# Ranks ahead of half of G, an earlier row table, two gathers in flight, and two weight loads held back, in a fused attention and two-MoE kernel

## What is computed

```python
# soft MoE: 32 slots, 4 for each of 8 experts
c = softmax(x @ phi, axis=1)                   # N x 32
x = c @ slot_out                               # slot_out is 32 x 512
# top-2 MoE
noisy = x @ w_gate + log1p(exp(x @ w_noise)) * noise
top2, top2_w = two best experts of each token, softmax of their two scores
for e in range(8):
    for k in range(2):
        rows = top2[:, k] == e
        h = np.maximum(x[rows] @ w1[e], 0.0)
        out[rows] += top2_w[rows, k, None] * (h @ w2[e])
```

## Time and profile before

| | |
|---|---|
| Median of 3 runs | 1070.62 us (1070.4 to 1071.17) |
| Profiled execution, its own time | 1072.71 us |
| Its span | 1070.9 us |
| Busy share of the span | PE 90%, DVE 73%, POOL 58%, ACT 57% |
| Chain that ended last, by engine | PE 31%, DVE 28%, issue 23%, POOL 6%, DMA 6%, ACT 3% |
| Mean DMA traffic | 98 GB/s |

### The profile page before, as it was taken

The page is one execution under the profiler, slowest core; times in us unless marked ns, Lnnn a source line. Parts: engine busy times, 40 slices in busy tenths (PEclk is TensorE's granted clock), DMA queues, the critical chain, the costliest instruction groups (busy, mean ns, idle before and its releaser), DMA issues.

```text
span 1070.9 us, 21707 instructions
## 1 busy us (share of the span) xinstructions
PE 962.8 (90%) x6439; PEld 674.3 (63%) x6439; DVE 785.2 (73%) x1511; ACT 612.2 (57%) x1243; POOL 621.4 (58%) x940
## 2 busy tenths in 40 slices
PE   3899998999999999999999989997699999999995
PEld 1566666666666666666666676332377878777884
DVE  5999999999999999999999963105735443554251
ACT  2787887787778878778878872102323332333121
POOL 3577777777777777777777760001444544555453
PEclk9999999999999999999999999998899999999998
DMA  9910110110110010010010006899915534433332
GB/s 349 421 46 34 47 30 15 45 45 12 33 45 12 33 45 12 33 45 21 24 45 12 0 1 229 329 420 422 384 22 120 120 42 113 117 42 41 43 41 32
DMA packets 23776, 105.14 MB, mean 98 GB/s; under 512 B 3200, under 2 KB 4288, under 8 KB 16576
## 3 DMA queue, kind: packets, MB, share of 16 engines
q1 hardware_dynamic: 15856, 84.54, 20.6%
q0 software_dynamic: 7168, 11.21, 8.0%
q10 hardware_dynamic: 720, 8.98, 2.3%
HBM read 88.39 MB, written 16.07 MB: 98 GB/s over the span
## 4 chain that ended last, share of the span: by engine, by line
PE 31%; DVE 28%; issue 23%; POOL 6%; DMA 6%; ACT 3%; DVEq 1%; SPq 1%; POOLq 0%; ACTq 0%
PE psum L843 14%; DVE arena L1049 8%; PE psum L848 7%; DVE arena L1045 6%; DVE arena L1037 5%; DVE arena L1033 3%; POOL arena L1334 3%; DMA arena<-w_top 2%; ACT h_hi L1009 2%; DVE arena L1053 2%; DMA arena<-xs_rows,arena 2%; POOL arena L1371 2%; DVE arena L1041 2%; PE psum L830 1%; PE psum L719 1%
## 5 line engine op out<-in xcount | busy, mean ns | idle before, releaser
L1334 POOL TENSOR_SCALAR arena<-arena 128x576 bf16<-128x576 f32 x144 | 249.5, 1733 | 135.5 <-DVE arena L1033 128.5
L586 PE MATMUL psum<-arena 128*128 128x130 f32 (+3 forms) x1600 | 220.6, 279 | 2.8 <-ACT arena L891 2.8
L586 PEld LDWEIGHTS psum<-arena 128*128 128x128 f32 (+3 forms) x1600 | 185.6, 178 | 35.7 <-ACT arena L891 3.3
L543 PE MATMUL psum<-arena 64*128 64x288 f32 (+1 forms) x640 | 111.8, 462 | 58.1 <-DVE arena L1041 53.1
L1293 DVE COPY arena<-psum 128x512 f32 x41 | 28.3, 691 | 152.9 <-PE psum L848 120.5
L843 PE MATMUL psum<-w_hi,h_hi 128*128 128x512 f32 x320 | 131.4, 411 | 6.5 <-ACT h_hi L1009 1.8
L871 ACT ACTIVATE arena<-arena 128x576 bf16<-128x576 bf16 x144 | 98.6, 685 | 64.6 <-POOL arena L1334 64.5
L1009 ACT ACTIVATE h_hi<-psum 128x512 fp32r<-128x512 f32 x80 | 43.4, 595 | 160.3 <-PE psum L830 159.5
L843 PE MATMUL psum<-w_lo,h_hi 128*128 128x512 f32 x320 | 126.9, 396 | 0.0
L1037 DVE MAX8 arena<-psum 128x8 f32<-128x576 f32 x144 | 109.3, 759 | 14.4 <-PE psum L555 13.3
L865 ACT COPY arena<-psum 128x576 f32<-128x576 f32 x144 | 90.6, 629 | 38.4 <-PE psum L543 38.1
(11 more groups left out here) (198 smaller groups left out, 1629.2 us busy)
## 6 DMA issues: line engine op xcount, KB each, us to landing
weights<-w_soft SPq DMA_DIRECT2D x21, 1024.0 KB, 16.1
arena<-qkv SPq DMA_DIRECT2D x15, 864.0 KB, 4.4
weights<-w_top SPq DMA_DIRECT2D x12, 1024.0 KB, 25.9
arena<-w_soft SPq DMA_DIRECT2D x11, 1024.0 KB, 9.5
weights<-w_top SPq DMA_DIRECT2D x3, 2048.0 KB, 26.6
weights<-w_top ACTq DMA_DIRECT2D x3, 2048.0 KB, 7.9
arena<-qkv SPq DMA_DIRECT2D x16, 325.0 KB, 2.9
out<-arena SPq DMA_DIRECT2D x1, 4864.0 KB, 18.3
```

What stands on the lines that cost most here:

```text
L543: last = nc.tensor.matmul(bank(2 * (t % 2) + x, SH)[q0:q0 + rows, :], qT[u][half, w * P + q0:w * P + q0 + rows], kT[u][half, h * SH:(h + 1 ...
L586: last = nc.tensor.matmul(o_place(n, k)[0:rows, :], wT[0:kr, t % 2, kc, q0:q0 + rows], v_, start=(kc == 0), stop=(kc == KC - 1))
L1334: nc.gpsimd.tensor_scalar(hit[t % 2], s_sb[t % S_SLOTS], m8[t % S_SLOTS][:, 7:8], None, ALU.is_ge) \
```

## The change

- PE: the rank matmuls move ahead of `g_part(0, 1)`. Reading the bounds moves from ahead of the L804 matmuls into `g_part(1, 1)`, two loads ahead of each of its four steps. `g_stack(4)` and `g_stack(5)` move from ahead of the loop into it: `g_stack(e + 4)` now follows experts 0 to 3.
- ACT: the write of the row table is issued after `g_high(0, 0)`. `g_out` of experts 0 to 3 goes ahead of `w2_high(0, 0)`. `w2_high(0, 1)` goes to POOL, as a copy, and `w2_high(1, 0)` goes behind the tiles of expert 0.
- DVE: takes `hi_hot`'s picked half and `w2_low(0, 0)` over from POOL. `w2_low(0, 0)` goes ahead of `c_low(1)`.
- POOL: the first gather has a semaphore of its own (`x_first`), and the second is issued without a wait for the first.
- SP: w2 of experts 2 and 3 is loaded only when both first gathers have landed.

```diff
@@ SP @@
             sp.wait_ge(g_ps, 2)
             for e in range(4):
+                if e == 2:
+                    sp.wait_ge(x_first, 16)
+                    sp.wait_ge(x_ready, 16)
                 load_w2t(sp, e)
@@ PE @@
-            def g_part(g, x):
+            def g_part(g, x, bounds=None):
...
                 for c in range(DC):
+                    if bounds is not None:
+                        bounds += [tile_bound(pe, 2 * c + 1), tile_bound(pe, 2 * c + 2)]
...
             g_part(0, 0)
-            g_part(0, 1)
 
             pe.wait_ge(st, 9)
...
+            g_part(0, 1)
             g_part(1, 0)
-            pe.wait_ge(rt_ready, 1)
-            bounds = tile_bounds(pe)
...
-            g_part(1, 1)
+            pe.wait_ge(rt_ready, 1)
+            bounds = [0]
+            g_part(1, 1, bounds)
...
-            for e in range(4, 6):
-                g_stack(e)
-            pe.wait_ge(w_lo_first, 1)
+            pe.wait_ge(g_lo, 4)
...
-                if e in (1, 2):
-                    g_stack(e + 5)
+                if e < 4:
+                    g_stack(e + 4)
@@ ACT @@
             g_high(0, 0)
+            act.wait_ge(rows_set, 1)
+            act.dma_start(xs_dram[0:ROWS, :].rearrange("(p a) r -> p (a r)", a=PICKS),
+                          rows_f).then_inc(tabled, 16)
             g_high(0, 1)
...
             g_high(1, 1)
+            for e in range(4):
+                g_out(e)
             w2_high(0, 0)
-            g_out(0)
-            g_out(1)
...
             x_copy(0, x_ring[:, 0:SL])
-            g_out(2)
-            g_out(3)
             c_high(1)
-            w2_high(0, 1)
             x_copy(1, x_ring[:, SL:2 * SL])
-            w2_high(1, 0)
...
+                if e == 0:
+                    w2_high(1, 0)
                 if e < E - 1:
                     w2_high(e + 1, 1)
@@ DVE @@
+            dve.wait_ge(hot_set, 1)
+            nc.vector.tensor_tensor(hi_hot[:, :, 0, :], col_hot,
+                                    cst[:, C_PICK:C_PICK + PICKS].unsqueeze(2).broadcast_to([P, PICKS, COLS]),
+                                    ALU.mult).then_inc(hot_hi, 1)
...
+            w2_low(0, 0)
             c_low(1)
             w2_low(0, 1)
@@ POOL @@
-            for n in range(2):
-                fetch(nowx[n], n, 0, idx_x, n)
-                if n > 0:
-                    pool.wait_ge(x_ready, 16 * n)
-                gather(n)
-            pool.wait_ge(w_hi, 1)
-            nc.gpsimd.tensor_tensor(w2_lo[0][:, 0:FC // 2, :], w2t_of(0)[:, 0:FC // 2, :],
-                                    w2_hi[0][:, 0:FC // 2, :].bitcast(F32), ALU.subtract).then_inc(w_lo_first, 1)
+            fetch(nowx[0], 0, 0, idx_x, 0)
+            gather(0, x_first)
+            fetch(nowx[1], 1, 0, idx_x, 1)
+            gather(1)
+            pool.wait_ge(g_ps, 4)
+            pool.wait_ge(w2t_in[0], 16)
+            nc.gpsimd.tensor_copy(w2_hi[0][:, FC // 2:FC, :], w2t_of(0)[:, FC // 2:FC, :]).then_inc(w_hi_pool, 1)
```

More of the change, by code:

```diff
@@ L314, in build @@
         pick_set = sem("pick_set")
-        hot_set, hot_dve, hot_act, hot_pool = sem("hot_set"), sem("hot_dve"), sem("hot_act"), sem("hot_pool")
+        hot_set, hot_dve, hot_act, hot_hi = sem("hot_set"), sem("hot_dve"), sem("hot_act"), sem("hot_hi")
         gate_set = sem("gate_set")
@@ L321, in build @@
         w2t_in = [sem(f"w2_top{s}") for s in range(4)]
-        x_ready, x_c = sem("x_ready"), sem("x_copied")
+        x_first, x_ready, x_c = sem("x_first"), sem("x_ready"), sem("x_copied")
         f_t = sem("f_t")
@@ L327, in build @@
         f_h, f_hc, f_lo = sem("f_h"), sem("f_hc"), sem("f_lo")
-        w_hi, w_lo, w_lo_first = sem("w2_hi"), sem("w2_lo"), sem("w2_lo_first")
+        w_hi, w_lo, w_hi_pool = sem("w2_hi"), sem("w2_lo"), sem("w2_hi_pool")
         f_y, f_yc = sem("f_y"), sem("f_yc")
@@ L838, in _ @@
                         if f % 4 == 0:
-                            if 2 * e + f // 4 > 0:
-                                pe.wait_ge(w_lo, 2 * e + f // 4)
+                            pe.wait_ge(w_lo, 2 * e + f // 4 + 1)
                             pe.wait_ge(f_hc, 2 * i + f // 4 + 1)
@@ L989, in x_copy @@
             def x_copy(n, slot):
-                act.wait_ge(x_ready, 16 * n + 16)
+                act.wait_ge(*((x_first, 16) if isinstance(n, int) and n == 0 else (x_ready, 16 * n)))
                 nc.scalar.copy(x_cur.rearrange("p (r s) -> p r s", r=4),
@@ L1019, in _ @@
                     g_out(e + 4, 2)
-            hold(act, x_ready, 16 * bounds[E] + 48)
+            hold(act, x_ready, 16 * bounds[E] + 32)
             hold(act, x_c, bounds[E] + 2)
@@ L1260, in w2_low @@
                 f = n * FC // 2
-                dve.wait_ge(w_hi, 2 * e + n + 1)
+                dve.wait_ge(*((w_hi, 1) if (e, n) == (0, 0) else (w_hi_pool, 1) if e == 0 else (w_hi, 2 * e + n)))
                 nc.vector.tensor_tensor(w2_lo[e % 4][:, f:f + FC // 2, :], w2t_of(e % 4)[:, f:f + FC // 2, :],
@@ L1415, in fetch, with gather @@
                 hold(pool, ready, count + 1)
-            def gather(slot):
+            def gather(slot, landed=x_ready):
                 nc.gpsimd.indirect_dma_start(
                     x_ring[:, slot * SL:slot * SL + SL], None, xs_dram[:, :], bass.IndirectOffsetOnAxis(ap=nowx[slot], axis=0),
-                    bounds_check=ROWS + P - 1, oob_is_err=True).then_inc(x_ready, 16)
+                    bounds_check=ROWS + P - 1, oob_is_err=True).then_inc(landed, 16)
             pool.sem_inc(out_free, 3)
@@ L1426, in _ @@
             pool.wait_ge(tabled, 16)
[L1427 to L1434 removed]
+            fetch(nowx[0], 0, 0, idx_x, 0)
[5 more added lines that the diff above has]
+            nc.gpsimd.tensor_copy(w2_hi[0][:, FC // 2:FC, :], w2t_of(0)[:, FC // 2:FC, :]).then_inc(w_hi_pool, 1)
             for n in range(2, AHEAD):
                 pool.wait_ge(x_c, n - 1)
+                if n == 2:
+                    pool.wait_ge(x_first, 16)
                 fetch(nowx[n % 2], n, 0, idx_x, n)
[L1438 removed]
+                pool.wait_ge(x_ready, 16 * n - 16)
                 gather(n % 2)
@@ L1448, in _ @@
                     fetch(nowx[k], 2 * i + k + AHEAD, 0, idx_x, 2 * i + k + AHEAD)
-                    hold(pool, x_ready, 32 * i + 16 * k + 16 * AHEAD)
+                    hold(pool, x_ready, 32 * i + 16 * k + 16 * AHEAD - 16)
                     gather(k)
@@ L1452, in _ @@
                     pool.sem_inc(out_free, 1)
-            hold(pool, x_ready, 32 * pairs + 16 * AHEAD)
+            hold(pool, x_ready, 32 * pairs + 16 * AHEAD - 16)
 def constants():
```

10 lines of the change are left out of this document (1 added, 9 removed).

## The result

| | before | changed |
|---|---|---|
| Median (lowest to highest) | 1070.61 us (1069.68 to 1071.17, 5 runs) | 1075.91 us (1074.44 to 1076.93, 5 runs) |
| Ratio, 95% interval | | 1.0049 [1.0034, 1.0064] |
| Profiled execution, its own time | 1072.71 us | 1074.75 us |
| Its span | 1070.9 us | 1072.9 us |

The change makes the kernel slower, by 5.3 us at the medians. The forecast was 1070.3 us, and its range ended at 1073.4. The two profiled executions are only 2.0 us apart, so the traces at hand explain less than half of it. That gap turned out to be the first lesson.

A forecast was written before the change was run, and what follows sets the result against it. It took waits between attention and the loop, mainly transfers, as the bound, with `g_part(1, 1)`'s weights remaining. 2.8 us won less 2.5 lost took 1072.71 to 1072.4, and the median 2.1 lower gave 1070.3 us; range 1066.2 to 1073.4.

The forecast's parts named there:

- The starting point: The forecast started from the profiled execution's 1072.71 us and put the median of the runs 2.1 us lower.
- the sum: Whole kernel: 2.8 us won, 2.5 us lost, so 0.3 us less, giving 1070.3 us at the median.
- The passage: Up to the loop's start: G ends at 762.7, loop starts at 771.6 instead of 774.65; gain 2.8 us.
- The third load: Before G's last part: weights of `g_part(1, 1)` land at 755.9 and PE, ready at 753.4, waits 2.5 us.
- The register loads: Before each step of G's last part: 0.5 us per load, two exposed for 1.0 us, the later ones hidden.
- Rival 3: Register loads in G's last part not hidden: G ends 3 to 5 us later, about 1074 us; chance 0.08.
- The gaps between experts: `h_hi` waits for stack and copy until T + 1.8, T ending an expert's last w2 matmul; 2.5 us lost.
- Rival 2: Between experts ACT comes out at T + 2.5: loss 5.5 us instead of 2.5, time 1073.3 us; chance 0.15.
- Part 3: The forecast's section on the gaps between experts, where stacks moved into the loop delay `h_hi`; 2.5 us lost.
- The page: The profile's DMA share was read as 90% or more in one stretch, about 670 to 770 us.
- Rival 1: Last G weights land before 753.4, or full clock and hidden loads: G ends 758.4 to 759.4, 1066.5 us; chance 0.27.

The follow-up runs named there:

- e4: The kernel before, unchanged, run and profiled a second time; median 1071.17 us, 1.0002 of before.
- e3: The kernel before with only stacks 4 and 5 moved into the loop, a stack following each of experts 0 to 3; 1076.36 us, 1.004 of before.
- e11: e5 with the row table written behind `hot_set` again; 1069.08 us, 0.9983 of before.
- e5: The changed kernel with stacks 4 and 5 and `w2_high(1, 0)` back ahead of the loop, and register loads ahead of the list matmuls; 1069.62 us.
- e0: The changed kernel, unaltered, run and profiled a second time; median 1075.04 us, 1.0045 of before.
- e13: The changed kernel, unaltered, profiled a third time; one run, 1075.12 us.
- e6: The changed kernel with w2 of experts 4 to 7 issued by SP, only after the gather under way has landed; 1076.02 us, 1.0053 of before.
- e2: The changed kernel with PE's eight register loads back ahead of the list matmuls; 1072.88 us, 1.0019 of before.

## Why the prediction was wrong

- **The starting point (wrong, about 2 us).** The step that failed is in the sum: "From the profiled execution's 1072.71 this gives 1072.4; the median of the runs stands 2.1 us lower, so **1070.3 us**." This takes the 2.1 us as lying outside the change. They lay inside: that execution had W at M + 50.6, e4 at M + 48.6, and e3, which up to there differs only by the two stacks, at M + 48.4. The waits that the change removed were in part waits that most runs don't have. Against the first profile the passage gained 2.6 us at W and 3.0 at S; against e4 it gained 0.6 and 1.4.
- **The passage, row by row (mostly right).** Ranks forecast for 736.3 came at 736.77; list matmuls 753.0 to 753.4, came by 754.2; weights 755.9, came 756.39; G ends 762.7, came 763.33; loop 771.6, came 772.21; w2 774.6, came 775.34. M itself was 0.47 us later. Forecast gain 2.8, measured 2.1, or 2.6 from M. DVE's three pieces without POOL took 5.09 us and the operation taken over 1.96, forecast 5.0 and 1.9. From G's end to the loop it was 8.88 us; 8.9 was forecast, though the terms given add up to 8.75. Both gathers had landed when ACT wanted them.
- **The third load (right).** "With the table in front at 755.9" has the right time. By e11 the table's new place has no part in it, since it is in front in the old place too; what its bytes cost stays open.
- **The register loads (right in kind, too small).** 1.0 us taken for the two exposed ones; 1.67 us measured from the landing to the first matmul, of which 0.14 us stands there without loads too (e5), so 0.8 us each. The six others are hidden, as forecast. Rival 3 didn't occur. The Trainium skill's floor of about 600 ns (DMA: Bandwidth & Descriptors, § Latency and other measured facts) gave 1.2 us and was nearer than the 0.5 us each that I took.
- **The gaps between experts (right, to 0.1 us).** 2.5 us forecast, with `h_hi` at T + 1.8. From the periods of boundary and first tiles: 0.91 + 0.08, 0.29, 0.27 and 0.91 + 0.09, together 2.55 us. Rival 2's size, T + 2.5, was not reached. (By its own rows its 5.5 us would be 5.3.)
- **What was left out (1.6 us and more).** This is the second step that failed: "**2.5 us lost**" takes the stacks' cost as ending with the expert's first tile. Part 3 asked what `h_hi` waits for in the first tile only. The gather of the second tile, POOL's scatter beside `w2_low`, and the 2 MB load were not followed. They cost 1.6 us in the changed kernel's profile, 1.5 in e0's, 2.2 in e13's, and more where the clock falls.
- **The page (misread, without effect).** Its DMA digits show 90% or more at 696 to 776 us, and in the first two slices, not at 670 to 770 us.
- **Rival 1 (did not occur).** It needed the last weights before 753.4. PE has them 29.1 to 29.5 us after M, with the early table and without it.

In sum: 0.3 us of gain was forecast. Against a typical run of before the passage gave 1.4 us to S, the loop lost 4.3 us, and the tail is 0.2 us longer: 3.2 us slower in e0. (The two executions are 4.0 us apart, but 0.8 of that is e0's later M, ahead of all that the change touches.) The medians differ by 4.2 (e0) to 5.3 us. The 1.0 to 2.1 us that remain lie in runs whose traces are not at hand, and their cause stays open.

## What to carry to other kernels

A wait in one profile may be that execution's own. If the profiled run lies off the median, find where, before a change is credited with removing that wait; a second profile of the kernel before would have taken about 2 of the 5.6 us of this error away. When work is moved out of a place where an engine idles anyway, its price in the new place includes everything queued behind it in order, and the phase in which the other engines now meet. And a shorter path can bring more than its own length: one reordering gave 3.4 us where the path through it promised 1.3, and 1.6 us of it was PE at a granted clock of 1.00 instead of 0.84.

## What the runs showed of the hardware

- A POOL indirect DMA instruction took 1.60 us beside an idle or later DVE, and 2.6 to 3.6 us when it started 0.1 to 1.2 us behind the start of DVE's pair of two-input subtractions (the changed kernel, e0, e3, e13); DVE's pair took 4.5 to 4.6 us in both cases. A copy of 128 x 1 numbers on POOL took 0.18 or 0.72 us, and up to 2.06 us beside that pair (before).
- A gather of 128 rows landed 7.2 to 8.3 us after its issue beside a 2 MB load (e0, e3, e13, before and the changed kernel), and within 3.6 us with none near it (884.79 for 881.19 in e6) and within 3.7 us with the load issued 2.05 us behind it (e2).
- 1.37 us of idle time on PE, in an otherwise dense loop, was followed by 3.4 us at half clock (e3), while 1.03 us in e0 and 1.32 us in e13, at the same place of a tile, left the granted clock at 1.00.
- DVE's three one-hot pieces (128 x 1536, bf16) took 7.98 us with POOL's two-input operation beside the first of them (before), and 5.09 us without it (the changed kernel).
